# Splitting GpSimd's low-part subtractions of the first expert layer into 256-column instructions

## What is computed

```python
# attention within chunks of 64 tokens, 4 batches x 8 heads x 576 x 64
attn = softmax(q_c @ k_c^T / sqrt(64));  x = (attn @ v_c) as [2304, 512]
# first expert layer, d_ff = 1536
x = ((x @ w_a) * (x @ w_b)) @ w_out
# second expert layer, d_ff = 2048
h = x @ w_in
g = (a0 + a1*h + a2*h^2 + a3*h^3) / (1 + |b0|*|h| + |b1|*h^2 + 1e-6)
out = g @ w_out2
```

## Time and profile before

| | us |
|---|---|
| median of 3 runs | 903.03 |
| lowest and highest | 902.39, 904.01 |
| the profiled execution's own time | 902.01 |
| its span, first to last instruction | 899.9 |
| TensorE busy | 883.8 |
| VectorE busy | 681.1 |
| ScalarE busy | 502.0 |
| GpSimd busy | 344.6 |

### The profile page before, as it was taken

How to read it: one execution, slowest core, us unless ns; L and a number is a source line. 1 busy time by engine, 2 the same in 40 slices (tenths; PEclk the granted TensorE clock), 3 DMA queues, 4 the chain that set the end, 5 groups by cost and what they waited for, 6 DMA issues and landing times.

```text
span 899.9 us, 14659 instructions
## 1 busy us (share of the span) xinstructions
PE 883.8 (98%) x5884; PEld 832.5 (93%) x5884; DVE 681.1 (76%) x886; ACT 502.0 (56%) x769; POOL 344.6 (38%) x297
## 2 busy tenths in 40 slices
PE   8999989899999999999999999999999999999998
PEld 7889879899999999999999998999999999999996
DVE  4667764667666666657655899998999899989887
ACT  4555652444444444445544677876666666666562
POOL 2120212888887778879875014200111011100000
PEclk9999999999999999999999999999999999999999
DMA  9975201222222222232211020002000200000002
GB/s 210 191 164 117 62 13 48 60 71 71 71 71 71 71 71 71 71 118 71 71 47 47 14 93 0 1 1 94 1 1 1 94 1 1 0 1 36 36 36 105
DMA packets 103235, 53.37 MB, mean 59 GB/s; under 512 B 58880, under 2 KB 94720, under 8 KB 103168
## 3 DMA queue, kind: packets, MB, share of 16 engines
q1 hardware_dynamic: 103168, 52.45, 21.5%
HBM read 47.71 MB, written 4.72 MB: 58 GB/s over the span
## 4 chain that ended last, share of the span: by engine, by line
PE 88%; DVE 5%; ACT 4%; SPq 2%; issue 1%; DMA 1%; DVEq 0%; ACTq 0%
PE ps L599 36%; PE ps L650 24%; PE ps L799 20%; PE ps L501 2%; SPq L314 1%; DVE tmp L1364 1%; PE ps L587 1%; PE ps L588 1%; PE ps L592 1%; PE ps L528 1%; PE ps L551 1%; DVE tmp L1370 1%; DMA y<-in_k 1%; PE ps L723 1%; PE ps L724 1%
## 5 line engine op out<-in xcount | busy, mean ns | idle before, releaser
L599 PE MATMUL ps<-x_hi,w 128*128 128x384 f32 x864 | 230.7, 337 | 0.6 <-DVE tmp L1383 0.3
L799 PE MATMUL ps<-w,g_hi 128*128 128x512 f32 x576 | 177.6, 391 | 0.0
L599 PEld LDWEIGHTS ps<-x_hi,w 128*128 128x128 f32 x864 | 157.1, 188 | 3.0 <-DVE tmp L1383 0.7
L599 PE MATMUL ps<-x_lo,w 128*128 128x384 f32 x432 | 144.7, 335 | 0.0
L458 POOL TENSOR_TENSOR w<-w 128x512 fp32r<-128x512 f32 x32 | 46.9, 1471 | 231.8 <-ACT w L917 231.8
L650 PE MATMUL ps<-x_hi,w 128*128 128x384 f32 x480 | 134.0, 334 | 1.5 <-DVE tmp L1251 1.5
L799 PEld LDWEIGHTS ps<-w,g_hi 128*128 128x128 f32 x576 | 107.4, 188 | 21.0 <-ACT g_hi L1111 0.4
L599 PE MATMUL ps<-g_hi,w 128*128 128x384 f32 x480 | 126.6, 334 | 0.0
L799 PE MATMUL ps<-w,g_lo 128*128 128x512 f32 x288 | 112.1, 392 | 0.0
L1241 DVE TENSOR_TENSOR y<-y,ps 128x384 f32<-128x384 f32 x120 | 65.7, 553 | 59.6 <-PE ps L599 59.6
L650 PE MATMUL ps<-w 128*128 128x384 f32 x540 | 103.4, 334 | 1.2 <-ACT ps L992 1.2
(11 more groups left out here) (122 smaller groups left out, 1660.6 us busy)
## 6 DMA issues: line engine op xcount, KB each, us to landing
w<-in_moe_w_out SPq DMA_DIRECT2D x32, 256.0 KB, 2.8
out<-y SPq DMA_DIRECT2D x18, 256.0 KB, 2.0
y<-in_q SPq DMA_DIRECT2D x16, 256.0 KB, 4.2
y<-in_k SPq DMA_DIRECT2D x16, 256.0 KB, 5.1
y<-in_v SPq DMA_DIRECT2D x16, 256.0 KB, 3.5
w<-in_moe_w_a SPq DMA_DIRECT2D x16, 256.0 KB, 3.1
w<-in_moe_w_b SPq DMA_DIRECT2D x16, 256.0 KB, 3.4
w<-in_moe_w_in SPq DMA_DIRECT2D x16, 256.0 KB, 4.0
```

What stands on the lines that cost most here:

```text
L599: last = nc.tensor.matmul(dst, left, right, start=n == 0, stop=n == 3 * len(pairs) - 1)
L799: last = nc.tensor.matmul(out_bank(n), left[:, 2 * (m % 2) + e, u * P:(u + 1) * P], w[:, slot2(fp), right, DC * HALF + e * D:DC * HALF + ( ...
```

## The change

In `rest_ws` the condition falls away: every n takes the pieces of 256 columns that n = 0 and 1 had. `rest_wo` makes two instructions of 256 columns of its one of 512; the second signals `wo_ready`. Semaphores and their counts stay as they are: the last piece of a cut signals `ws_ready`. So 28 quads go from 3 to 7 instructions and 30 quads from 1 to 2: 142 more instructions on GpSimd. The number of columns that are subtracted is the same.

```diff
                 for i, (at, to) in enumerate(W_CUTS):
                     pool.wait_ge(ws_hi_done, 3 * n + i + 1)
-                    pieces = [(at, to)] if n >= 2 else [(c, c + HALF) for c in range(at, to, HALF)]
-                    for start, stop in pieces:
+                    for start, stop in ((c, c + HALF) for c in range(at, to, HALF)):
                         last = nc.gpsimd.tensor_tensor(w[:, w_slot(n), LO, start:stop], raw_w(n, start, stop),
                                                        w[:, w_slot(n), HI, start:stop], ALU.subtract)
                     last.then_inc(ws_ready, 1)
 
             def rest_wo(n):
                 pool.wait_ge(wo_hi_done, n + 1)
-                nc.gpsimd.tensor_tensor(w[:, w_slot(n), LO, WO:SLOT], raw_w(n, WO, SLOT), w[:, w_slot(n), HI, WO:SLOT],
-                                        ALU.subtract).then_inc(wo_ready, 1)
+                for start, stop in ((WO, WO + HALF), (WO + HALF, SLOT)):
+                    last = nc.gpsimd.tensor_tensor(w[:, w_slot(n), LO, start:stop], raw_w(n, start, stop),
+                                                   w[:, w_slot(n), HI, start:stop], ALU.subtract)
+                last.then_inc(wo_ready, 1)
```

## The result

The changed kernel takes 900.51 us (median of 10 runs, 899.07 to 902.11) against 902.88 us (902.13 to 905.15, 10 runs) for the kernel before. The ratio is 0.9979 with a 95% interval of 0.9970 to 0.9989: 1.9 us faster, between 1.0 and 2.7. The prediction was 1.7 us. As a time it was 901.3, in a range of 900.6 to 904.0: the median itself lies 0.1 us under that range, but over its ten runs the kernel before came to 902.88 and not 903.03, and 903.03 times the ratio is 901.1.

A forecast was written before the change was run, and what follows sets the result against it. TensorE was taken as the bound, with only its wait for VectorE's L1251 in block 0 to win. Of that stall's 1.76 us, 1.7 was taken, GpSimd's added 19.9 at nothing: 903.03 - 1.7 = 901.3, range 900.6 to 904.0.

The forecast's parts named there:

- The bound: Whole kernel: TensorE, busy 883.8 of 899.9 us; a GpSimd change helps only where TensorE waits for it.
- the two waits: TensorE, 141 to 500 us: 1.5 us for VectorE's L1251, winnable; 1.2 us for ScalarE's L992, which stays.
- The stall: Block 0: TensorE waits for L1251 behind three long VectorE instructions; L1251 was to start at 164.0 instead of 165.78.
- The price of 1.76: Block 0: TensorE's stall for L1251 with its restart costs 1.76 us, of which 1.7 was taken as won.
- rest_ws(2): GpSimd, block 0: would give VectorE three turns and end at 165.1 in place of 163.09.
- The cover for w_out1's low parts: GpSimd, block 0: done at 168.5, wanted by second_sum at 168.91; cover 0.4 us.
- rest_ws(3): GpSimd, ahead of quad_head(3): transfer for sums(4) 4.3 us, done at 180.7, due at 181.4; cover 0.7 us.
- rival B: First blocks: thin covers fail, GpSimd late once or twice; 0 to 1.7 us given back, middle 902.2; chance 0.18.
- GpSimd's round: GpSimd's loop of loads, sums and low parts: 22.3 us against TensorE's 22.88 for a block, so it keeps up.
- GpSimd's busy time: Whole kernel: the added instructions cost 19.9 us, raising it from 344.6 to about 364 us.
- VectorE's waits: VectorE behind GpSimd: at most 0.70 us in place of 1.25 or 1.8; L1263's mean from 803 to about 650 ns.
- Rival C: GpSimd gives no turn between short pieces, VectorE waits for all seven, nothing won: 903.0 to 903.6; chance 0.10.

The follow-up runs named there:

- e2: Kernel before, with rest_ws and rest_wo in pieces of 256 columns everywhere but block 0, which keeps whole cuts; ratio to before 1.0002.
- e4: Kernel before, with only GpSimd's cut of 768 columns split, into 512 and 256, everything else whole; ratio to before 0.9988.
- e1: Kernel before, with pieces of 256 columns only up to block 0, whole cuts later; ratio to before 0.9995.
- e3: Kernel before, GpSimd unchanged; in block 0 alone VectorE makes the next pair's first input sums after corners(1) and rest_g(1); ratio to before 0.9992.
- e9: Kernel before, with pieces of 256 columns through blocks 0 and 1, whole cuts from block 2 on; ratio to before 0.9987.
- e12: Kernel before, GpSimd in whole cuts; in all blocks VectorE makes the next pair's input sums after corners and rest_g; ratio to before 0.9977.
- e13: Kernel before, VectorE's input sums moved later in all blocks and ScalarE's casts reordered in block 0; 898.64 us against 902.12, ratio 0.9960.
- e5: Changed kernel, with pieces of 128 columns from n = 2 on and in all of rest_wo; 925.04 us, ratio to the kernel before 1.0255.

## Why the prediction was right, point by point

- **The bound.** That only the two waits of the earlier trace rows could be won, and the second not by this change: right but for 0.10 at 418 us (see e2), where the trace was taken to be without a gap.
- **The stall.** Predicted from L1263's start to L1251's start 164.0 - 160.08 = 3.9 us; measured 163.33 - 159.49 = 3.84. The price of 1.76, restart included, was the measured one. (One reading was off: GpSimd's first instruction for w_out1 is recorded to end at 165.05, not 165.16, so L1281 ended 0.81 behind it, as L1279 had.)
- **rest_ws(2).** Predicted 165.1 - 158.46 = 6.64 us long; measured 6.63. The cover for w_out1's low parts was to be 0.4; it is 168.33 - 167.61 = 0.7.
- **rest_ws(3): the term that was mis-sized.** The cover was to be 0.7 and was gone. The chain of work shows the stage from head(3) on with 0.24 more than 10.40, and the weight loads name GpSimd:

```profile
180.98 10.64 PE ps L651 x60
```

```profile
PEld ps L651 <- POOL w L446: 0.3, 1, 0.3
```

  The transfer for sums(4) was costed at 4.3 us behind rest_ws(2), as before; it took 169.52 - 164.50 = 5.0. The second piece went out 0.80 behind rest_ws(2)'s end in both kernels, but took 4.2 us to land and not 3.4; quad 3's loads follow it 2.3 us later and not 3.9. That the two slow each other is likely and not shown. So rival B did happen, by 0.24, where I had set 0.05. The sum of the stretch is 1.75 - 0.24 + 0.10 (the small gap at 418 us, also gone) = 1.61, as measured. That the 0.10 I had not seen made up for part of the 0.24 is luck.
- **GpSimd's round.** Predicted 22.3 us; the first is 203.00 - 180.82 = 22.18, the first five have a mean of 22.4 (one of them 23.14), then it is TensorE's own 22.88. It does keep up. The last three are longer, 24.57, 23.25 and 23.18, 2.4 us over in sum; that takes from the cover there, but TensorE does not wait.
- **GpSimd's busy time.** Predicted 364, measured 375.7. The 19.9 of pieces are right (an undisturbed run is 4.90 us), but 11 us more are turns given to VectorE: the time by which GpSimd's sums and low parts last longer than undisturbed ones rose from some 27 to 40 us in sum. (That number is an estimate from the durations in both traces.)
- **VectorE's waits.** L1263's mean was to fall from 803 to 650 ns. The groups of VectorE, 150 to 480 us, beside the earlier trace rows:

```profile
L1264 DVE TENSOR_TENSOR g_lo<-tmp,g_hi 128x384 fp32r<-128x384 f32 x58 | 44.2, 762 | 16.3 <-ACT g_hi L1013 12.6
...
L1299 DVE TENSOR_TENSOR w<-x_hi,w 128x768 f32<-128x768 f32 x2 | 3.0, 1495 | 0.0
```

  762, and L1298, which took 0.95 before, takes 1.49 now. Shorter waits, but more of them: 36 of the 58 took over 0.6 us, where 21 of 57 had. A GpSimd that works for more of the time makes more of the two-input instructions wait. VectorE's busy time fell by only 4 us (681.1 to 677.1). I had priced the one wait that mattered and taken the others to shrink with it; none of them is on the path.
- **Rival C** (no turn between short pieces) is out: e4 and the changed kernel show a turn after each instruction.
- **What the prediction did not see:** that block 0 alone would not be enough. The sum said 1.7 for a stall in one place, and for the whole change that was right, but e1, e3 and e9 show that the pieces behind block 0, which I costed as a mere burden, carry the gain through blocks 1 and 2. So the size was right for the whole change with a reason that covers block 0 alone; in e1 the same reasoning was off by half.

That the median fell by a little more than the stretch (1.9 by the ratio, 2.4 by the medians, 1.61 in the stretch) is inside the interval.

## What to carry to other kernels

A wait that stands in one place of the profile can be the first of a row: the next one shows only when the first is gone, so look at the places behind it that have the same instructions and ask how much room they had. Where two engines exclude each other, the length of one instruction sets the other's wait, but cutting it up also costs the first engine time and gives its idle time away; moving the victim out from ahead of the instruction for which TensorE waits gained the same here for nothing (e12), and left room for the next improvement (e13).

## What the runs showed of the hardware

VectorE's instructions with two SBUF inputs and GpSimd's took turns, one instruction each, wherever the timelines above show both at work, at 768, 512, 256 and 128 columns: VectorE's 768 columns take 2.60 us behind an instruction of 768, 2.04 behind 512, 1.49 behind 256 and 1.21 behind 128 (e5, L1290), where 0.95 is undisturbed. The wait itself (1.65, 1.1, 0.54, 0.26) is about 0.15 us less than the time from start to start of GpSimd's instructions (1.80, 1.25, 0.70, 0.42). So 0.15 us of one engine's instruction overlap with the other's; whether it is the start of VectorE's or the end of GpSimd's is not shown. The instructions of VectorE that have one input in PSUM, L1251, L1254, L1256 and L1258, took 0.54 to 0.56 us in every kernel. "SBUF — State Buffer" of the Trainium skill, section "Who interferes with whom", says this for pairs of instructions; the runs add the turn-taking and its size.
